# Attention on one core: the tensor engine's loop over chunks written out, three products cut into halves and quarters of 64 rows

## The reference

```python
# batch 4, heads 8, 768 tokens, head size 48, all float32
k_n = k / (norm(k) + 1e-6)
for t in range(S):
    y[:, :, t] = q[t] @ state                       # state is 48 x 48 per head
    v_old = k_n[t] @ state
    state = state + beta[t] * outer(k_n[t], v[t] - v_old)
x = y as 3072 rows of 384                           # then:
# a mixture of 8 experts, each row to the expert of its largest logit: relu(x @ w1[e]) @ w2[e], times the gate
# a dense layer: elu(x @ w_in) @ w_out, with w_in 384 x 2048
```

## Time and profile before

| | us |
|---|---|
| median of 3 runs | 1100.64 |
| profiled execution | 1103.74 |
| its span | 1102.0 |
| PE busy | 967.5 |
| DVE busy | 630.4 |
| ACT busy | 586.7 |
| attention, from the start to the last product of L426 | about 396 |
| L381, busy as MATMUL over the whole run | 62.4 |
| L329, the same | 63.5 |
| L426, the same | 53.3 |

### The profile page before, as it was taken

One profiled execution on the slowest core, in us unless ns is written; L12 is line 12 of the kernel. 1 busy time (PEld: TensorE's weight loads), 2 busy tenths in 40 slices (PEclk: granted clock), 3 DMA queues, 4 the chain that ended last, 5 costly groups with the idle time before them and its releaser, 6 DMA issues. The chain is left out here.

```text
span 1102.0 us, 25678 instructions
## 1 busy us (share of the span) xinstructions
PE 967.5 (88%) x10563; PEld 673.8 (61%) x10563; DVE 630.4 (57%) x1106; ACT 586.7 (53%) x1141; POOL 259.2 (24%) x303
## 2 busy tenths in 40 slices
PE   1798998989899884069999999999999999999996
PEld 0587887878788752046666667655555555555553
DVE  5678686868678546356665654244444444444442
ACT  2566574747477552346666664354545454454542
POOL 6556463646256111710000000000101001010101
PEclk9989897979799977589999999999999999999998
DMA  6022132312122001774555541000000000000000
GB/s 215 16 81 86 43 102 66 91 55 77 43 69 63 2 1 53 241 252 145 150 155 151 151 155 47 1 1 1 29 1 29 1 1 29 0 29 0 29 1 29
DMA packets 38108, 74.05 MB, mean 67 GB/s; under 512 B 3817, under 2 KB 29553, under 8 KB 38001
## 3 DMA queue, kind: packets, MB, share of 16 engines
q1 hardware_dynamic: 34928, 63.05, 18.5%
q0 software_dynamic: 3072, 9.45, 2.3%
HBM read 63.04 MB, written 9.45 MB: 66 GB/s over the span
## 5 line engine op out<-in xcount | busy, mean ns | idle before, releaser
L1406 PE MATMUL bankH<-rows_or_y,wd 128*128 128x512 f16 (+1 forms) x864 | 201.8, 379 | 1.6 <-PEq L1045 1.6
L1418 PE MATMUL bankO<-wd,gd_hi 128*128 128x384 f16 x768 | 187.4, 326 | 0.6
L1406 PEld LDWEIGHTS bankH<-rows_or_y,wd 128*128 128x128 f16 x864 | 84.5, 98 | 93.5 <-issue 1.7
L665 DVE CAST_PREDICATED merge<-pair_mask,bankA 128x512 f16<-128x512 uint16 x144 | 100.5, 698 | 56.1 <-PE bankA L346 55.9
L1418 PE MATMUL bankO<-wd,gd_lo 128*128 128x384 f16 x384 | 125.2, 326 | 0.0
L534 ACT CAST x_inv<-bankA 128x512 f16<-128x512 f32 x120 | 70.4, 587 | 86.2 <-PE bankA L357 86.2
L1418 PEld LDWEIGHTS bankO<-wd,gd_hi 128*128 128x128 f16 x768 | 74.6, 98 | 62.1 <-DVE gd_lo L1480 2.8
L1503 POOL DMA_INDIRECT out<-o_rows,dest x24 | 25.6, 1069 | 346.7 <-ACT o_rows L1457 290.4
L1473 DVE SCALAR_TENSOR_TENSOR gd<-hd_exp,hd 128x512 f32<-128x512 f32 x96 | 66.5, 692 | 66.8 <-ACT hd_exp L1443 66.8
L1480 DVE SCALAR_TENSOR_TENSOR gd_lo<-gd,gd_hi 128x512 f16<-128x512 f32 x96 | 66.5, 692 | 64.4 <-ACT gd_hi L1451 64.4
L1451 ACT ACTIVATE gd_hi<-gd 128x512 f16<-128x512 f32 x96 | 60.4, 630 | 69.1 <-DVE gd L1473 69.0
(11 more groups left out here) (187 smaller groups left out, 1791.5 us busy)
## 6 DMA issues: line engine op xcount, KB each, us to landing
kq_t<-in_kq_rows SPq DMA_DIRECT2D x24, 512.0 KB, 4.6
stage<-in_moe_w SPq DMA_DIRECT2D x24, 512.0 KB, 3.6
stage<-in_moe_w SPq DMA_DIRECT2D x32, 384.0 KB, 3.6
rows_or_y<-x_sorted SPq DMA_DIRECT2D x12, 385.0 KB, 7.4
k_norm<-in_k_tok SPq DMA_DIRECT2D x24, 192.0 KB, 2.4
v_in<-in_v_tok SPq DMA_DIRECT2D x24, 192.0 KB, 2.4
k_tok<-in_k_tok SPq DMA_DIRECT2D x24, 192.0 KB, 3.5
stage<-in_moe_w_in SPq DMA_DIRECT2D x8, 384.0 KB, 3.2
```

Of the source, the lines that this page charges most:

```text
L665: nc.vector.copy_predicated(half_cols(merge[:, i], i, False), pair_mask[:, i, :].rearrange("p (n b) -> p n b", b=2 << i).unsqueeze(1) .to_ ...
L1406: last = nc.tensor.matmul(h_bank[f % 4][:, :], wd1[:, a, c, P * f:P * f + P], y_t[:, b, c, bass.ds(blk * NB, NB)], start=c == a == b == 0, ...
L1418: last = nc.tensor.matmul(o_bank[s][:, 0:DM], (g_lo if a else g_hi)[:, f % 4, P * s:P * s + P], wd2[:, b, f, :], start=f == a == b == 0, s ...
```

## The change

1. The loop is gone: the tensor engine's program is written out for all 24 items, as that of the other engines.
2. `times_state` and `within_chunk` issue each product as two, one for output rows 0 to 63 and one for 64 to 127: the weights are 64 columns wide instead of 128, the moving operand is the same.
3. `gram` issues each product as two quarters (48 rows by 64 columns of weights). The half with output rows 0 to 63 still has 2 x 128 columns; the half with rows 64 to 127 has only 2 x 64, columns 64 to 127 of each block, since the others are masked. The part that is no longer written is set to zero once, by two memsets of the vector engine at the start.

```diff
-def over_items(eng, body):
-
-    for b in range(-GRAM, B):
-        body(Item(0, b))
-    with eng.Fori(1, NCH - 1) as c:
-        for b in range(B):
-            body(Item(c, b))
-    for b in range(B):
-        body(Item(NCH - 1, b))
...
                 for p in range(2):
-                    for e in range(2):
-                        ps = slice(DP * e, DP * e + D)
-                        last = nc.tensor.matmul(pair_bank[e][:, 256 * p:256 * p + 256], kq_t[ps, it.b, 2 * r + p, 0, :],
-                                                kq_t[ps, it.b, 2 * r + p, :, :].rearrange("p a i -> p (a i)"),
-                                                start=True, stop=True)
+                    for f in range(2):
+                        for e in range(2):
+                            ps = slice(DP * e, DP * e + D)
+                            half = slice(DP * f, DP * f + DP)
+                            to = pair_bank[e][half, 256 * p:256 * p + 256].rearrange("p (a i) -> p a i", a=2)
+                            last = nc.tensor.matmul(to[:, :, DP * f:P], kq_t[ps, it.b, 2 * r + p, 0, half],
+                                                    kq_t[ps, it.b, 2 * r + p, :, DP * f:P], start=True, stop=True)
...
                 for p in range(NP):
-                    last = nc.tensor.matmul(to[:, 2 * D * p:2 * D * p + 2 * D], kq_t[:, it.b, p, a, :],
-                                            state[:, it.b, p].rearrange("p e d -> p (e d)"),
-                                            start=p == 0, stop=stop, skip_group_check=True)
+                    for f in range(2):
+                        half = slice(DP * f, DP * f + DP)
+                        last = nc.tensor.matmul(to[half, 2 * D * p:2 * D * p + 2 * D], kq_t[:, it.b, p, a, half],
+                                                state[:, it.b, p].rearrange("p e d -> p (e d)"),
+                                                start=p == 0, stop=stop, skip_group_check=True)
...
                 for h in range(H):
-                    last = nc.tensor.matmul(out_bank[:, D * h:D * h + D], bt_pt[:, it.b, h, 1, :], u[:, h, :],
-                                            start=False, stop=True, skip_group_check=True)
+                    for f in range(2):
+                        half = slice(DP * f, DP * f + DP)
+                        last = nc.tensor.matmul(out_bank[half, D * h:D * h + D], bt_pt[:, it.b, h, 1, half], u[:, h, :],
+                                                start=False, stop=True, skip_group_check=True)
...
-            over_items(pe, body)
+            each_item(-GRAM, body)
...
             nc.vector.memset(state[:], 0.0)
+            for e in range(2):
+                nc.vector.memset(pair_bank[e][:, :], 0.0)
```

More of the change, by code:

```diff
@@ L38, in exists @@
     def exists(self):
-        return not isinstance(self.n, int) or 0 <= self.n < NT
+        return 0 <= self.n < NT
 def need(eng, sem, value):
```

## The result

The changed kernel took 1062.12 us, the median of 4 runs (1059.92 to 1064.11), against 1100.76 for the kernel before (4 runs, 1093.97 to 1103.78): a ratio of 0.966 (95% interval 0.961 to 0.971), 38.6 us. The profiled execution took 1064.11 us against 1103.74.

What follows compares the result with a forecast made beforehand. The prediction took PE to pace each attention item, with DVE close behind. Loop 7.7, items 12.4 and low-clock stretches 2.0 summed to 22 us, giving 1079 us against the median, with 8 in 10 between 1066 and 1094.

Steps and rivals of the forecast that it cites:

- What bounds an item, and the stalls: Attention stage: PE paces an item of 12.77 us, DVE close behind; the four waits at L635 remain.
- The loop, 7.7 us: Tensor engine's loop in attention: writing it out removes three turns, costing 7.7 us together.
- the turn of the last round: Last jump back of the tensor engine's loop, priced at 20.91 - 17.74 = 3.17 us.
- the last chunk: Attention's final items, 12.49 us each without key norms to sum; taken as support that straight-line fetching keeps pace.
- The halves and quarters: PE products per item: output 0.63 us less, keys 0.15, queries 0.05, each gram round 0.05; 0.93 in sum.
- the fourth rival: Split products: halves run one after the other, slower than before, giving 1134 us; chance 0.04.
- What the item keeps: Attention item: L339's wait for L658 leaves 0.54 us of 0.93, period 12.23; 12.4 us over 23 intervals.
- the first rival: Attention item: all 0.93 us is kept, 9 us more, giving 1070; chance 0.12.
- The clock: Stretches at 1.2 GHz after the L635 waits: still about 13.6 us each, extra saving 2.0 us in all.
- the extra at 0.5 a stretch: Added saving of the split products within each of four stretches at 1.2 GHz, 2.0 us together.
- The memsets: Two vector-engine memsets at the start: delay well under 2 us, hidden by GpSimd's 8.71 us wait for k_norm.

Runs made afterwards that it cites:

- e1: Kernel before with only the tensor engine's loop written out, all products whole: 1091.65 us, ratio 0.992 to the kernel before.
- e9: Changed kernel with the output product running all 8 heads' upper halves first, then all lower ones: 1079.72 us, ratio 0.977 to the kernel before.
- e10: Changed kernel with a 128x64 vector-engine memset just ahead of the copy the transpose waits for: 1061.61 us, ratio 0.962 to the kernel before.
- e12: Changed kernel with the seventh norm step ahead of the solution step and the eighth behind the state update: 1048.69 us, ratio 0.950 to the kernel before.
- e2: Kernel before, loop kept, with state and output products in halves and gram products whole: 1079.84 us, ratio 0.981.
- e3: Kernel before with the loop written out and only the output product in halves: 1070.23 us, ratio 0.971.
- e13: Kernel before, loop written out, whole products, seventh norm step ahead of the solution step, eighth behind the state update: 1064.00 us, ratio 0.967.
- e5: Kernel before with the loop written out and only the gram products in quarters, with their memsets: 1085.06 us, ratio 0.982.
- e6: Changed kernel with only the seventh norm step moved ahead of the solution step: 1059.31 us, ratio 0.962 to the kernel before.

## Why the prediction was wrong, step by step

- **What bounds an item, and the stalls.** Right: PE paces the item, and the four waits at L635, now L631, stayed, with an idle of 2.5 us at each.
- **The loop, 7.7 us.** Right for the idle: items 12.77 in e1, no idle for issue, and 9 us (6 to 12) in all. Incomplete in the reading: the turn of the last round was priced at 3.17 us because its idle fell into a stretch that was longer than the others; the clock's share was counted as the turn's. And a support that was misread: the items at 12.49 us were taken for written-out ones of the last chunk, but the loop's third and last turn, at 296.81, starts its round for chunk 4, and the items from 310.23 on belong to it, so they ran inside the loop. Written-out items at full pace were only the first ones, 12.77 us from 67.89; e1, with 12.77 and 12.49 throughout, settles what the misread items could not.
- **The halves and quarters.** Right to 0.02 us each: 0.64 for 0.63, 0.14 for 0.15, 0.05 for 0.05. All four quarters ran side by side, and the fourth rival (halves in turn) did not happen, but e9 shows it is real for neighbours in the same half. The Trainium skill (TensorE: Matmul & The Clock Gate, Part 3) says that loads overlap products only across row groups; L422's 32 MATMULs in 1.14 us, 0.058 us a pair on the same rows, differ, and the measurement decides.
- **What the item keeps: the step that was mis-sized.** I took L658's 1.21 us from the one item in the earlier trace rows. The very next item of the same trace has it at 0.73:

```profile
201.06 0.73 DVE L658 COPY_PREDICATED y_inv<-next_mask,bt_hi 128x512 f16<-128x512 uint16 x1
```

  Both items took 12.77 us, since before the change nothing waited for it. In the traces of the two kernels it is 0.73 to 0.76 where it starts 0.01 to 0.02 us ahead of GpSimd's operation, and 1.20 to 1.25 where it starts 0.01 to 0.06 behind; in the ordinary items of the changed kernel it was ahead, up to the last norm steps. That the order is the cause is not shown: in e10 the copy took 0.67 us from behind, and one copy of e12 (at 147.16) took 1.27 from 0.01 us ahead. Behind the last norm steps, in the items that the forecast calls the last chunk, it took 1.23, and there the forecast's arithmetic holds:

```profile
299.22 0.62 PE L331 MATMUL bankA<-ident,y_inv 128*128 128x128 f16 x8 [0.32 <-DVE y_inv L654]
```

  The transpose started 2.37 us after the L338 at 296.85 (2.35 forecast), after a wait of 0.32 (0.4 forecast), and the item took 11.95 where it had taken 12.49: 0.54 kept, exactly the forecast. In the 16 items ahead of these the first rival, that the output product's whole saving is kept, is what happened: 0.81 instead of 0.54, 0.27 x 16 = 4.3 us.
- **The clock: the step that failed.** "I put the extra at 0.5 a stretch, four times 2.0", and "each followed by about 13.6 us at 1.2 GHz". The stretches shrank to 3.4 to 6.8 us, worth some 14 us in the profiled executions where 2.0 were put. I had treated their length as a constant of the chip because three of four were alike. The evidence against it was in the trace: the fourth had 17.1 (0.38 x 20.91 x 2 = 15.9 of it in the item of the earlier trace rows), and it was the one whose turn cost 3.17. I used that as a price and not as a sign that the length can change. Of the 17.5 us between the forecast's 22.1 and the 39.6 of the two profiled executions, 12 are this. The loop's turns inside the stretches are one part (e1, e2), the halves another (the count above, and e3 against e1), and the idle ahead of them is what each stretch needs at all (e12, e13); what ends a stretch stays open.
- **The memsets** show no cost at the end, as forecast: the first output product came 2.1 us earlier. e5, which has them too and the same 10.2 us at 1.2 GHz ahead of that product as the kernel before, has it at 68.24, 0.35 later.

## What to carry to other kernels

Small float32 products paced by their weight loads are worth cutting into column halves if the neighbours in the program lie in different halves; alternate them product by product. Before a saving is followed to a wait, read the awaited instruction in every item, not in one. Time at the low clock at the norm steps followed idle times of 1.7 us and more here, and its length changed with the kernel: count what a change does to it, over several executions, since single stretches scatter from 3.4 to 13.7 us. Look first for the idle: moving two small vector steps out of the way of GpSimd's long operation brought a further gain a third as large as this whole change.

## What the hardware showed unexpectedly

- Four quarters of the array (48 rows by 64 columns, float32) run at once: four MATMULs start within 30 ns, and 16 with 256 columns take 1.03 us, where 8 of whole width took 1.07.

```profile
196.47 0.43 PE L322 MATMUL bankA<-kq_t 48*64 48x256 f32 x4
```

- In the changed gram round the last product issued is a narrow one, with half the columns to stream; in the trace it ends at 197.14. The vector engine, idle and waiting for its increment, started at 197.69, 0.14 us after the wide ones had ended (196.47 + 1.08) [the timeline above]: the increment did not run ahead of products issued earlier on other quarters.

```profile
197.69 0.69 DVE L644 TENSOR_TENSOR bt_pt<-bankA,maskb 128x512 f32<-128x512 f32 x1 [0.55 <-PE bankA L322]
```

- The idle of 2.5 us brought the granted clock to 1.2 GHz at all four places of every kernel that had it; 1.84 us in e6 did so at two of four, 1.74 us in e12 at its one place; the idle of 0.64 us did not at any of seven places in e12 and e13.
- The quarters in a loop were not tried, nor was what exactly PE must do for a low stretch to end.
